# Attention in 32-row blocks against 64 keys: sixteen full steps and four leftover steps in place of twenty-four

## The reference

```python
scores = (q @ k.T) / sqrt(64)              # q, k, v: 4 batches, 8 heads, 576 positions, 64
rel = pos[:, None] - pos[None, :]
mask_local = (rel >= 0) & (rel < 32)                  # heads 0 to 3
mask_strided = (rel >= 0) & (pos_k % 32 == pos_q % 32)  # heads 4 to 7
scores = where(mask, scores, -1e9); scores -= max(scores, -1)
attn = exp(scores); attn /= sum(attn, -1) + 1e-9
x = attn @ v            # then rows (batch, position) by 512 columns, for the two later stages
```

## Time and profile before

| | us |
|---|---|
| median of 3 runs | 704.72 (703.4 to 707.56) |
| the profiled execution | 707.21 |
| its span, first to last instruction | 705.4 |
| attention: first masks to first logit matmul | 5.57 to 91.94 |

### The profile page before, as it was taken

The page is one execution under the profiler, slowest core; times in us unless marked ns, Lnnn a source line. Parts: engine busy times, 40 slices in busy tenths (PEclk is TensorE's granted clock), DMA queues, the critical chain, the costliest instruction groups (busy, mean ns, idle before and its releaser), DMA issues.

```text
span 705.4 us, 11023 instructions
## 1 busy us (share of the span) xinstructions
PE 657.4 (93%) x4149; PEld 567.2 (80%) x4149; DVE 328.2 (47%) x614; ACT 229.2 (32%) x693; POOL 149.7 (21%) x163
## 2 busy tenths in 40 slices
PE   7999891299999999889999999999999999999995
PEld 4887761299999999868888888888888888888994
DVE  3877632041111112466545654456444564455653
ACT  4999932031111111122223322233222332222331
POOL 2565606302222222884000200002000020000201
PEclk9999977599999999989999999999999999999998
DMA  8555176692777775331000100001000010000100
GB/s 261 181 208 212 34 283 245 238 404 87 272 269 271 268 259 186 89 106 43 1 1 0 61 1 0 1 0 59 0 0 0 0 60 0 0 0 1 61 1 30
DMA packets 37854, 73.95 MB, mean 105 GB/s; under 512 B 2739, under 2 KB 16224, under 8 KB 37808
## 3 DMA queue, kind: packets, MB, share of 16 engines
q1 hardware_dynamic: 34936, 63.92, 26.4%
q0 software_dynamic: 2880, 9.52, 3.5%
HBM read 63.49 MB, written 9.94 MB: 104 GB/s over the span
## 4 chain that ended last, share of the span: by engine, by line
PE 83%; ACT 6%; POOL 2%; DMA 2%; issue 2%; DVE 2%; SPq 1%; DVEq 0%
PE pair L969 28%; PE pair L982 15%; PE bank L982 12%; PE pair L927 11%; PE bank L937 10%; ACT prob L489 5%; POOL x_sorted L418 2%; DMA k_str<-kT 1%; PE bank L841 1%; PE bank L911 1%; PE bank L827 1%; PE bank L868 1%; ACT XT L497 1%; PE pair L814 1%; DVE yl L747 1%
## 5 line engine op out<-in xcount | busy, mean ns | idle before, releaser
L572 ACT ACTIVATE cl<-cl,half 128x512 f32<-128x512 f32 (+1 forms) x80 | 54.5, 681 | 190.2 <-DVE cl L768 190.2
L477 POOL DMA_INDIRECT out<-XT,tok x18 | 18.8, 1045 | 355.5 <-DVE XT L756 351.6
L776 DVE TENSOR_TENSOR gl<-gr,gh 128x512 fp32r<-128x512 f32 (+1 forms) x80 | 54.5, 681 | 73.6 <-ACT gh L581 72.4
L768 DVE TENSOR_SCALAR cl<-pair 128x512 f32<-128x512 f32 (+1 forms) x80 | 50.9, 637 | 74.9 <-PE pair L969 74.7
L969 PE MATMUL pair<-yl,WIH 128*128 128x512 f32 (+1 forms) x320 | 81.0, 374 | 2.5 <-DVE yl L747 2.5
L969 PE MATMUL pair<-yh,WIH 128*128 128x512 f32 (+1 forms) x320 | 79.8, 371 | 1.3 <-ACT yh L548 1.3
L969 PE MATMUL pair<-yh,WIL 128*128 128x512 f32 (+1 forms) x320 | 79.6, 371 | 0.0
L927 PE MATMUL pair<-xw,WE 128*128 128x168 f32 x512 | 75.5, 309 | 0.0
L927 PEld LDWEIGHTS pair<-xw,WE 128*128 128x128 f32 x512 | 74.4, 192 | 0.1
L581 ACT CAST gh<-gr 128x512 fp32r<-128x512 f32 (+1 forms) x80 | 46.3, 579 | 85.6 <-PE bank L982 59.6
L937 PE MATMUL bank<-hid,WE 128*128 128x168 f32 x512 | 74.1, 306 | 0.0
(11 more groups left out here) (124 smaller groups left out, 932.6 us busy)
## 6 DMA issues: line engine op xcount, KB each, us to landing
WE<-w SPq DMA_DIRECT2D x16, 2048.0 KB, 9.2
xrow<-x_sorted SPq DMA_DIRECT2D x6, 781.5 KB, 10.9
raw_in<-win SPq DMA_DIRECT2D x16, 256.0 KB, 9.5
raw_out<-wout SPq DMA_DIRECT2D x16, 256.0 KB, 2.6
v_loc<-vl SPq DMA_DIRECT2D x4, 768.0 KB, 5.2
q_str<-qT SPq DMA_DIRECT2D x4, 576.0 KB, 5.8
k_str<-kT SPq DMA_DIRECT2D x4, 576.0 KB, 7.0
q_loc<-qT SPq DMA_DIRECT2D x3, 576.0 KB, 5.3
```

The costliest lines, as they stand in the source:

```text
L477: pool.indirect_dma_start(out, bass.IndirectOffsetOnAxis(tok[:, GT * g + t:GT * g + t + 1], 0), rows_of(g, t), None).then_inc(out_done if ...
L572: act.activation(cl[:, 0:n], cl[:, 0:n], ACT.Square, bias=half[:, :], scale=0.5).then_inc(squared, 1)
L768: dve.tensor_scalar(cl[:, 0:n], h2_b[f % 2][:, 0:n], -1.0, 1.0, ALU.max, ALU.min).then_inc(clamped, 1)
L776: dve.tensor_tensor(gl[:, f % 2, 0:n], gr[:, 0:n], gh[:, f % 2, 0:n].bitcast(F32), ALU.subtract).then_inc(g_low, 1)
```

## The change

The tiles become smaller units that are packed into full 128-row tiles. A local unit is a block of 32 queries against 64 keys (the block before and its own), four of which fill a tile's 128 rows. A strided unit is a strip of three classes (54 queries against the same 54 keys), two of which stand in a tile at rows 0 and 64. Each tile keeps 64 score columns per head, so a step holds 128 x 512 scores in place of up to 96 x 1024. A step is still two tiles for four heads. A batch has four full steps (strided, strided, local, local) and leaves over two local blocks, two strips and a narrow third strip of 36. The leftovers of a batch are one more step, and the four leftover steps run after all full steps of all batches: 20 steps, in the order 16 and 4.

On the engines the following moves. `exps` is one instruction over 128 x 512, since VectorE now subtracts the maximum itself (L656 of the changed kernel) and sums the rows (L662). The copy of the transposed weights goes from VectorE to ScalarE (L537). The result is one pair of banks in place of two banks in turn, and `place` makes two copies for a strided step, one for a local one, three for a leftover one. GpSimd multiplies once per step. TensorE still has its loop over batches; the other engines' rounds are written out. SP loads queries, keys and values step by step in place of batch by batch, and the leftovers of all batches in fewer, strided transfers.

```diff
-CLASSES = [6, 6, 5, 5, 5, 5]
...
+
+
...
+STRAIGHT = [
+    (strided_tile(0), strided_tile(2)),
+    (strided_tile(4), strided_tile(6)),
+    (local_tile(0), local_tile(4)),
+    (local_tile(8), local_tile(12)),
+]
+REST_OF_BATCH = (
+    (MASK_S, [(0, strided(8)), (64, strided(9))]),
+    (MASK_X, [(0, local(BLOCKS - 2)), (BLOCK, local(BLOCKS - 1)), (64, strided(STRIPS - 1))]),
+)
+TB = len(STRAIGHT)
+STEPS = B * TB + B
...
-LAG = 3
+SLOTS = 4
+LAG = FIRST = 3
+LOOPS = (B * TB - FIRST) // TB
```

The three parts of the loads, the work of GpSimd and ScalarE, and that of VectorE:

```diff
+            for i in range(TB):
+                load_qk(0, i)
+            for i in range(TB):
+                load_v(0, i)
+            for n in range((B - 1) * TB):
+                b, i = divmod(n, TB)
+                sp.wait_ge(scored, n + 1)
...
+                    sp.wait_ge(pv_done, n - LAG + 1)
+                    load_v((n - LAG) // TB + 1, (n - LAG) % TB)
```

```diff
                 pool.wait_ge(inverted, n + 1)
-                for j in range(2):
-                    q, kk, _, _, _, _ = TWINS[i][j]
-                    pr = prob[0:q, i % 3, 0:8 * kk].rearrange("q (h j p k) -> q h j p k", h=2, j=2, p=2)[:, :, j]
-                    inv = sm[0:q, i % 3, 24:32].rearrange("q (h j p) -> q h j p", h=2, j=2)[:, :, j]
-                    pool.tensor_tensor(pr, pr, inv.unsqueeze(3).to_broadcast([q, 2, 2, kk]), ALU.mult).then_inc(normed, 1)
-
-            steps(pool, step, 1)
-
-            pool.wait_ge(turned, 2 * STEPS)
+                weights = prob[:, n % SLOTS, :].rearrange("q (g k) -> q g k", g=8)
...
         @block.scalar
         def _(act):
-            def exps(n, i):
-                q, kk, _, _, _, _ = TWINS[i][0]
-                act.wait_ge(biased, n + 1)
-
-                behind(act, turned, 2 * (n - 2))
-                for e in range(8):
-                    last = act.activation(prob[0:q, i % 3, e * kk:(e + 1) * kk], score_b[i % 2][0:q, e // 4, e % 4 * kk:(e % 4 + 1) * kk], ACT.Exp,
-                                          bias=sm[0:q, i % 3, 8 + e:9 + e], scale=SCALE, accum_out=sm[0:q, i % 3, 16 + e:17 + e])
-                last.then_inc(probs_done, 1)
-
-            def place(n, i, b):
-
+            def exps(n):
+                act.wait_ge(lowered, n + 1)
+                act.activation(prob[:, n % SLOTS, :], prob[:, n % SLOTS, :], ACT.Exp, scale=SCALE).then_inc(probs_done, 1)
+
+            def copy_turned(n):
+                act.wait_ge(turned, n + 1)
+                behind(act, pv_done, n - 1)
+                act.copy(probT[:, n % 2, :], probT_b[n % 2][:, :]).then_inc(turn_copied, 1)
+
+            def place(n):
+                i, b = step_of(n)
                 act.wait_ge(pv_done, n + 1)
-                dst, src = x_place(i, b)
-                act.copy(dst, src).then_inc(x_placed, 1)
-
-            def step(k, s, b):
-                if not (isinstance(s, int) and s >= STEPS):
-                    exps(s, k % TB)
-                m = s - LAG
-                if not (isinstance(m, int) and m < 0):
-                    place(m, (k - LAG) % TB, b + (k - LAG) // TB)
-
-            steps(act, step, LAG)
...
+                if i < 2:
+                    act.copy(x_strided(b, 12 * i, 6), out_b[:, 0, 0:4 * STRIP].rearrange("d (p r m) -> d p r m", p=2, m=PHASE))
+                    act.copy(x_strided(b, 12 * i + 6, 6), out_b[:, 1, 0:4 * STRIP].rearrange("d (p r m) -> d p r m", p=2, m=PHASE)).then_inc(x_placed, 1)
+                elif i < TB:
...
+            for s in range(STEPS + LAG):
+                if 0 <= s - 1 < STEPS:
+                    exps(s - 1)
+                if 0 <= s - LAG < STEPS:
+                    copy_turned(s - LAG)
+                    place(s - LAG)
 
```

```diff
+            def maxima(n):
+                small, scores = sm[:, n % SLOTS], score_b[n % 2][:, :, 0:256].rearrange("q h (g k) -> q h g k", g=4)
                 dve.wait_ge(scored, n + 1)
-
-                behind(dve, probs_done, n - 2)
-                dve.tensor_reduce(sm[0:q, i % 3, 0:8], score_b[i % 2][0:q, :, 0:4 * kk].rearrange("q h (e k) -> q h e k", e=4), AX_X, ALU.max, negate=True).then_inc(maxed, 1)
+                behind(dve, normed, n - SLOTS + 1)
+                dve.tensor_reduce(small[:, 0:8].rearrange("q (h g) -> q h g", h=2), scores, AX_X, ALU.max).then_inc(maxed, 1)
                 dve.wait_ge(maxed, n + 1)
-                dve.tensor_scalar(sm[0:q, i % 3, 8:16], sm[0:q, i % 3, 0:8], SCALE, None, ALU.mult).then_inc(biased, 1)
...
+                behind(dve, turned, n - SLOTS + 1)
+                dve.tensor_tensor(prob[:, n % SLOTS, :].rearrange("q (h g k) -> q h g k", g=4, h=2), scores,
+                                  small[:, 0:8].rearrange("q (h g) -> q h g", h=2).unsqueeze(3).to_broadcast([P, 2, 4, KEYS]), ALU.subtract).then_inc(lowered, 1)
+
+            def inverses(n):
+                small = sm[:, n % SLOTS]
                 dve.wait_ge(probs_done, n + 1)
-                dve.tensor_scalar(sm[0:q, i % 3, 16:24], sm[0:q, i % 3, 16:24], 1e-9, None, ALU.add).then_inc(summed, 1)
+                dve.tensor_reduce(small[:, 8:16], prob[:, n % SLOTS, :].rearrange("q (g k) -> q g k", g=8), AX_X, ALU.add).then_inc(summed, 1)
                 dve.wait_ge(summed, n + 1)
...
-            def copy_turned(n, i):
-                behind(dve, pv_done, n)
-                for j in range(2):
-                    q, kk, _, _, _, _ = TWINS[i][j]
-                    dve.wait_ge(turned, 2 * n + j + 1)
-                    dve.tensor_copy(probT[0:kk, j, 0:4 * q], probT_b[j][0:kk, 0:4 * q]).then_inc(turn_copied, 1)
...
+                dve.tensor_scalar(small[:, 16:24], small[:, 8:16], 1e-9, None, ALU.add).then_inc(guarded, 1)
+                dve.wait_ge(guarded, n + 1)
+                dve.reciprocal(small[:, 24:32], small[:, 16:24]).then_inc(inverted, 1)
```

TensorE:

```diff
             def scores(n, i, b):
-                qs, ks, arrived = (q_str, k_str, qk_str_in) if i >= LB else (q_loc, k_loc, qk_loc_in)
-                if i % LB == 0 and not (isinstance(n, int) and n == 0) or isinstance(n, int) and n == 1:
-                    pe.wait_ge(arrived, 32 * (b + 1))
-
-                behind(pe, probs_done, n - 1)
-                s = score_b[i % 2]
-                for j in range(2):
-                    q, kk, _, _, strided, t = TWINS[i][j]
-                    mask = mask_b[0:q, (C_MS - C_ML0 if strided else P if t else 0):][:, 0:kk]
+                if i < TB:
+                    pe.wait_ge(qk_in[i], 32 * (b + 1))
+                elif b == 0:
+                    pe.wait_ge(qk_rest_in, 16 * 8)
+                behind(pe, lowered, n - 1)
+                out = score_b[i % 2 if i < TB else n % 2]
+                for hh in range(2):
+                    for j, (mask, _) in enumerate(tiles_of(i)):
+                        pe.matmul(out[:, hh, 0:256].rearrange("q (p j k) -> q p j k", p=2, j=2)[:, :, j], ident_b[:, :], mask_b[:, mask, :].unsqueeze(1).to_broadcast([P, 2, KEYS]),
+                                  start=(j == 0), stop=False, skip_group_check=True)
+
+                for j, (_, strips) in enumerate(tiles_of(i)):
+                    for p in range(2):
+                        for row, (kind, t, q) in strips:
+                            for hh in range(2):
+                                queries, keys = operands(i, b, p, slice(64 * hh, 64 * hh + 64), kind, t, q)
+                                col, width = P * p + 64 * j, q if kind == "s" else KEYS
+                                last = pe.matmul(out[row:row + q, hh, col:col + width], queries, keys, start=False, stop=(j == 1 and p == 1), skip_group_check=True)
+                last.then_inc(scored, 1)
...
+            def turn(n, i):
+                par, slot = (i % 2, i) if i < TB else (n % 2, n % SLOTS)
+                pe.wait_ge(normed, n + 1)
+                for g in range(4):
+                    last = pe.transpose(probT_b[par][:, P * g:P * (g + 1)], prob[:, slot, P * g:P * (g + 1)], ident)
+                last.then_inc(turned, 1)
...
+            def values(n, i, b):
+                if i < TB:
...
+                pe.wait_ge(turn_copied, n + 1)
...
+                pairs_ = list(itertools.zip_longest(*(strips for _, strips in tiles_of(i))))
+                for p in range(2):
                     for hh in range(2):
-                        pe.matmul(s[0:q, hh, 2 * j * kk:2 * (j + 1) * kk].rearrange("q (p k) -> q p k", p=2), ident_b[0:q, 0:q], mask.unsqueeze(1).to_broadcast([q, 2, kk]),
-                                  start=(j == 0), stop=False, skip_group_check=True)
-
-                for j in range(2):
-                    q, kk, q0, k0, _, _ = TWINS[i][j]
-                    for p in range(2):
-                        for hh in range(2):
-                            half_ = slice(64 * hh, 64 * hh + 64)
-                            last = pe.matmul(s[0:q, hh, (2 * j + p) * kk:(2 * j + p + 1) * kk], qs[half_, p, q0:q0 + q], ks[half_, p, k0:k0 + kk],
```

(79 more changed lines are left out.)

238 lines of the change are left out of this document (135 added, 103 removed).

## The result

The changed kernel takes 713.36 us (median of 4 runs, 711.59 to 715.22) against 705.3 for the kernel before beside it (4 runs): a ratio of 1.0115, 95% interval 1.0085 to 1.0145. It is slower by 1.2%: inside the forecast's range, but a loss where a gain was forecast. An execution more than 1.5% above the fastest of its kernel counts as slow and is left out of the ratios in this document, but not out of the medians, so a ratio need not be the quotient of two medians. The profiled execution has a span of 711.6 us at a mean granted clock of 0.936; before they were 705.4 and 0.963.

What follows compares the result with a forecast made beforehand. ACT was taken to bind narrowly, PE right behind. Start 13.0, 20 rounds 72.7 and last place 0.8 gave 86.5 against 91.9: 5.4 us saved, 701.8 from the profiled 707.2, 699.3 in medians; range 688 to 714.

Steps and rivals of the forecast that it cites:

- The step that failed: SP's loads in the attention rounds: 2 to 6 issues of some 0.4 us each, ready three rounds ahead, costed at nothing.
- the sign of it: What late loads would show in the trace: SP's transfers ahead of the score matmuls in the waits, a local step's first.
- The start: Start of the attention: first transposes at 13.0 us, where before the strided keys held the pipeline to 15.9.
- The ring of 14.8 us per batch: Chain through ACT's place, exponential and copy, then PE's values: four rounds of 3.12, 3.40, 4.29 and 4.01 us.
- Values: PE's value matmuls, set by their weight loads: 1.07 us in a strided step, 1.96 in a local one.
- The rival of cheap records: Value weight loads hide behind the other tile's matmuls: values 0.9 and 1.0 us, 15.5 saved, 689 us; chance 0.22.
- Floor: No PE record starts sooner than 25 ns after the last: 5 us more, 704, no gain; chance 0.18 including small waits.
- present record cost: Each PE score or value record keeps costing 36 ns: batches of 18.8 us, net 10.6 slower, 715; chance 0.13.
- The clock: Rival: PE's waits and short records bring half clock, about 2 us more per round affected; 714 us; chance 0.12.
- The sum: Attention's end: first turn at 13.0, 20 rounds of 72.7 together, last place 0.8, giving 86.5 against 91.9 us.

Runs made afterwards that it cites:

- start_act: Changed kernel with the twelve first transfers of V (batch 0) issued by ScalarE instead of SyncE; 710.7 us, ratio 1.0114 to the kernel before.
- v_packed: Changed kernel with V laid out in device memory so that each step's part is one transfer, not four or two; 699.5 us, ratio 0.9904 to the kernel before.
- copy_first: v_packed with ScalarE copying the turned probabilities before it takes the next step's exponentials; 698.9 us, ratio 0.9899 to the kernel before.
- warm_tail: v_packed with two dense matmuls ahead of the values in each of the last six rounds; 696.1 us, ratio 0.9855 to the kernel before.
- tiny_64: v_one_short plus 32 extra SyncE transfers, each of 64 rows of 8 bytes; 713.0 us, ratio 1.0088 to the kernel before.
- half_bytes: Changed kernel with as many issues, but half the bytes in Q, K and V transfers from batch 1 on; 733.0 us, a time that cannot be used.
- v_one_short: Changed kernel with one transfer of V per step as in v_packed, but strided V in the old 1 KB rows; 701.2 us, ratio 0.9875.
- all_packed: Changed kernel with one transfer for Q and K and one for V per step, two for all leftovers; 696.2 us, ratio 0.9822 to the kernel before.
- tiny_1: v_one_short plus 32 extra SyncE transfers, each of one row of 8 bytes; 702.5 us, ratio 0.9949 to the kernel before.
- combined: all_packed with the dense matmuls of warm_tail and the ScalarE order of copy_first; 694.6 us, ratio 0.9824 to the kernel before.

## Why the prediction was wrong

- **The step that failed:** "SP issues 2 to 6 loads per round, some 0.4 us each, and has each ready three rounds ahead; ... so about 350 could be had. I cost them at nothing." All three parts were off. An issue right behind others takes 0.6 us. The kernel before shows both prices, 0.6 in the run at its start and 0.36 to 0.38 later, with pauses between:

```profile
2.60 0.61 SPq L264 DMA_DIRECT2D q_loc<-qT  x1
3.25 0.61 SPq L265 DMA_DIRECT2D k_loc<-kT  x1
...
35.21 0.36 SPq L264 DMA_DIRECT2D q_loc<-qT  x1
35.66 0.38 SPq L265 DMA_DIRECT2D k_loc<-kT  x1
```

The loads were not ready three rounds ahead: SyncE issues in order and was hardly ever free between 1 and 71 us. The twelve transfers of batch 0's V (8.3 us) stood before batch 1's Q, but start_act shows that this block alone isn't the loss. And the rate at a full share was 266 to 280 GB/s (36 to 48 and 60 to 70 us). Against v_packed, step 2 came 4.8 us later after its predecessor, 7 and 8 together 4.5, 9 to 11 6.3, 12 to 15 3.0 (2.2 of it in step 15, a stall without a wait); with 0.3 at the start, 0.1 in step 3, and 1.3 and 0.5 the other way in steps 1 and 4 that makes the 17.3 us at step 15. Half clock has its share in this: the local values at 40.18 and 60.16 us last 2.44, those at full clock 1.46. The prediction did name the sign of it, but thought that a local step's scores would wait first; the strided K did.

- **The start** was right: first transposes at 12.4 (forecast 13.0).
- **The ring of 14.8 us per batch** was too long: 11.8 where nothing waits for a load. Values take 1.44 us and not 1.96, and copy_first shows that ScalarE's order matters little. The rival of cheap records was the right one for PE's side: v_packed's first logit matmul came at 78.6, where that rival gave 86.5 - 10 = 76.5.
- **Floor and present record cost** were wrong. 64 local score records go from first to last start in 0.64 us, 10 ns each. By the Trainium skill (TensorE: Matmul & The Clock Gate, "Wait — 56ns, not 53.3ns?") start to start never drops below about 25 ns; for small tiles side by side the trace contradicts it, for whole phases now and not only for the logits.
- **The clock** fell as its rival said, but as a second cost: v_packed, which hardly waited for loads, had 0.93 from 12 to 60 us, the changed kernel 0.78. From step 15 to the first logit matmul the changed kernel takes 21.7 us, v_packed 16.6, warm_tail 16.2: 5 us of the loss. Before the fall PE had waited (busy 5.6 of 12 us from 48 on, stalls of 0.7 and 2.6 us at 71 and 76).
- **The sum:** forecast for the attention's end 86.5; the first logit matmul came at 101.0. That is v_packed's 78.6, 17.3 for the loads and what followed from them, and 5.1 for the half clock. The parts are those of two executions, and v_packed's was its fastest; in the medians loads and clock together are 13.9 us.

The Trainium skill names what the profile showed (Perfetto Trace Analysis, "What 'DMA-bound' means"): a kernel can be bound by the issuing engine's sequencer, seen as a track solid with DMA slices, and those slices are the making of descriptors, not the moving of data. Here SPq is nearly solid from 1 to 71 us, and tiny_64 agrees. The issue of 3.27 us, 0.51 in half_bytes, does not fit a slice that is the making of descriptors alone.

**Open:** how the changed kernel's loss divides between issuing and the DMA engines' rate (half_bytes removed 11 us up to step 15 at the same number of issues; its issues got shorter too, 0.63 to 0.48 us, and start_act's earlier issues won 0.8); what decides whether the clock is full or half in the leftovers' rounds; and whether the stalls without a wait are instruction fetches. v_one_short's runs spread over 691 to 707 us, at mean granted clocks of 0.961 down to 0.935.

## What to carry to other kernels

When a change cuts a step's input into more transfers, count the issues on the queue, take 0.6 us for each of 64 rows or more in a run of them, and lay them end to end over the whole loop: here their sum mattered, and taking one block of twelve off the queue did not help (start_act). A DMA share read at few transfers says nothing of the rate with many. Laying the data out so that a step is one transfer of Q and K and one of V turned 1.2% slower into 1.8% faster, with the order of the work untouched.

## What was not expected of the hardware

- The time of an issue went with its rows and not with its bytes up to 64 rows: 0.35 us for 1 row, 0.48 for 32, 0.63 for 64, at 8 bytes a row (tiny_64) as at 1 KB (the changed kernel). Beyond that it grew no more: 0.61 for the 256 rows of Q or K, 0.50 to 0.61 for the 512 of the leftovers' Q and K (27.3 to 29.6 us). Behind a pause it was 0.33 (all_packed) and 0.33 to 0.38 (the kernel before in its steady state). Right behind transfers of one row (tiny_1) V's transfers of 128 or 256 rows took 0.36 to 0.41, and the Q behind them 2.15: an issue's time depends on what stands ahead of it too.
- Issues on ScalarE took 0.5 to 1.1 us, and held back its exponentials and the copies behind them by up to 2.9 us.
- PE's clock stayed at the lower of its two levels (1.2 GHz, granted 0.50) while PE was busy 10 of 10 us (80 to 90 in the changed kernel) and 17 of 18 (combined, with two dense matmuls in a round). In warm_tail it stayed at the upper one, at 12.3 of 14.
